# One mask per pair of heads, and VectorE's state scan and output addition placed ahead of the second decay scan

## The chip, the core and the metric

The kernel runs on one core of a Trainium2 chip. The metric is the device time of one launch in microseconds, the median of the runs. The engines named here are TensorE (PE in the profile, its weight loads PEld), VectorE (DVE), ScalarE (ACT), Pool (POOL) and SyncE (SP), which issues the loads. Each works through its own queue in order; semaphores tie the queues together.

## What is computed

Attention with a decaying state, then two mixtures of experts. Only the first part is touched by the change:

```python
def _attn_ref(r, k, v, w, u):             # r, k, v, w: 4 x 8 x 768 x 48
    state = np.zeros((B, H, D, D))
    for t in range(S):
        kt, vt, rt, wt = (k[:, :, t], v[:, :, t], r[:, :, t], w[:, :, t])
        cur = np.einsum('bhd,bhe->bhde', u[None] * kt, vt)
        y[:, :, t] = np.einsum('bhd,bhde->bhe', rt, state + cur)
        state = wt[:, :, :, None] * state + np.einsum('bhd,bhe->bhde', kt, vt)
```

Its output, 3072 rows of 384, goes through a top-1 mixture of 8 experts (`moe_`) with a skip gate, and that result through a second one with slots (`moe2_`).

## The kernel before

The attention runs over 16 pairs of heads (`PAIRS`), two heads side by side in the 128 partitions. A pair's 768 steps are cut into 6 chunks (`NC`) of 128 columns (`C`). Inside a chunk the recurrence becomes a product of scaled inputs: r and k are multiplied by running products of w counted from the middle of the chunk, their scores are masked to earlier steps, and only the states between chunks are carried.

The queues of one pair n, in their order:

- VectorE: `mid_up` (L1215), a scan over half of w; `products`: a reciprocal (L1221), `mid_w` (L1222, five numbers per partition, what each chunk leaves of the state) and the second scan (L1226, `mid_down`); `x_out(n - 3)` (L1260), which adds output and bonus of an earlier pair and frees the output bank `y_cols`; `k_input(n)` (L1240); `chain(n - 1)` (L1253), the scan that carries the states from the chunk sums in PSUM; `r_inputs(n)`: the r product (L1244) and `rk` (L1247).
- TensorE: transposes of k (L543, the fifth chunk at L546), first group of scores `a_products(n, 0)` (L572, two chunks of both heads), bonus rows (L554), second and third group of scores, transposes of the output of pair n - 2 (L605), transposes of the bonus rows (L561), chunk sums (L581), and the output products of pair n - 1 (L593 from the state, L598 from the masked scores).
- ScalarE: spreads `mid_w` over the columns (L1033), copies the output (L999), k (L991, L993), the first scores (L1016), the bonus rows (L1004), the second and third scores, the bonus (L1008), and multiplies v by it in 12 small instructions (`weigh_v`, L1026).
- Pool: three masks (L1586), one per group of scores, 512 columns each, as soon as ScalarE has copied the group.
- SyncE: loads of w, r, k and v, three pairs ahead (L430 to L441).

What ties them: the transposes of k wait for `k_input(n)` and for `chain(n - 1)` (L541); the first scores for the r product; `chain(n)` for the chunk sums of n (L1250) and for the spread middle weights; the output products for the state, for the output bank freed by `x_out` (L589), and for the masks (L595). A group of scores waits for the copy of the group two before it, since there are two buffers. The bonus rows lie in `a_bank`, beside the scores (L345).

Of the kernel before, what the change touches and what calls it, by code (L numbers as in the profile page):

```python
# [11 lines left out]
ACT = mybir.ActivationFunctionType  # L12


def build(nc, wrk, vt, ublock, sizes, w_skip, w_gate, w1, w2, phi, e1, e2, out):
    B, H, S, D = sizes
    P = 128
# [29 lines left out]
    with ctx:  # L47
# [294 lines left out]
        WHOLE = HALF  # L342
        y_cols = y_bank[:, :, :].rearrange("p b t -> p (b t)")[:, 0:S]

        def bonus_cols(g):  # L345

            return a_bank[:, 2 * (g % 2), 2 * C:4 * C]


        def half_rows(t, h0, h1, backwards):  # L350
# [179 lines left out]
        def _(pe):  # L530
# [15 lines left out]
                nc.tensor.transpose(sums_bank[:, NC * D:NC * D + C], k_in[:, c * C:(c + 1) * C], ident[:, :]).then_inc(ktok_full, 1)  # L546

            def bonus_rows(n):
                out = bonus_cols(3 * n + 1)
                if n:  # L550
                    pe.wait_ge(a_copied, 3 * n)
                for c in range(NC):
                    i = c % 4
                    last = nc.tensor.matmul(out[32 * i:32 * i + 32, c // 4 * C:(c // 4 + 1) * C], u_sb[:, n % QP, :], rk[:, c * C:(c + 1) * C],  # L554
                                            start=True, stop=True, tile_position=(0, 32 * i), skip_group_check=True)
                last.then_inc(bonus_full, 1)
# [7 lines left out]
            def a_products(n, s):  # L564
                g = 3 * n + s
                if g >= 2:
                    pe.wait_ge(a_copied, g - 1)
                for c in (2 * s, 2 * s + 1):
                    cols = slice(c * C, (c + 1) * C)
                    for a in range(2):  # L570
                        rows = slice(64 * a, 64 * a + 64)
                        last = nc.tensor.matmul(a_bank[:, 2 * (g % 2) + a, (c % 2) * C:(c % 2 + 1) * C], k_in[rows, cols], r_in[n % 3][rows, cols],  # L572
                                                start=True, stop=True, tile_position=(64 * a, 0), skip_group_check=True)
                last.then_inc(a_full, 1)
# [11 lines left out]
            def y_products(n):  # L586
                pe.wait_ge(state_ready, n + 1)
                if n:
                    pe.wait_ge(y_free, n)  # L589
                for c in range(1, NC):  # L590
                    for a in range(2):
                        rows = slice(64 * a, 64 * a + 64)
                        nc.tensor.matmul(y_cols[64 * a:64 * a + D, c * C:(c + 1) * C], state[n % 2][rows, :, c - 1], r_in[n % 3][rows, c * C:(c + 1) * C],  # L593
                                         start=(c in (1, 4)), stop=False, tile_position=(64 * a, 64 * a), skip_group_check=True)
                pe.wait_ge(a_masked, 3 * n + 3)  # L595
                for c in range(NC):
                    for a in range(2):
                        last = nc.tensor.matmul(y_cols[64 * a:64 * a + D, c * C:(c + 1) * C], v_sb[n % 4][:, c, a, :], a_sb[n % 2][:, a, c, :],  # L598
                                                start=False, stop=True, tile_position=(0, 64 * a), skip_group_check=True)
                last.then_inc(y_full, 1)  # L600

            def y_transposes(n):
                pe.wait_ge(y_copied, n + 1)
                for c in range(NC):
                    last = nc.tensor.transpose(y_cols[:, c * C:(c + 1) * C], y_ch[:, c * C:(c + 1) * C], ident[:, :])  # L605
                last.then_inc(y_turned, 1)
# [5 lines left out]
            for n in range(PAIRS):  # L612
                k_transposes(n)
                pe.wait_ge(r_ready, n + 1)
                a_products(n, 0)
                pe.wait_ge(rk_ready, n + 1)
                bonus_rows(n)
                a_products(n, 1)
                a_products(n, 2)
                if n >= 2:  # L620
                    y_transposes(n - 2)
                pe.wait_ge(ktok_copied, 2 * n + 1)
                bonus_turned(n)
                chunk_sums(n)
                if n:
                    y_products(n - 1)

# [358 lines left out]
        def _(act):  # L986
# [13 lines left out]

            def copy_bonus_rows(n):
                act.wait_ge(bonus_full, 2 * n + 1)
                act.wait_ge(a_full, 3 * n + 2)
                nc.scalar.activation(bonus_ch, bonus_cols(3 * n + 1), ACT.Copy).then_inc(bonus_copied, 1)  # L1004

            def copy_bonus(n):
                act.wait_ge(bonus_full, 2 * n + 2)
# [26 lines left out]
                                     ACT.Copy).then_inc(mid_rows_ready, 1)  # L1034

            act.wait_ge(tables_begun, 2)
            for t, n in ((sums_bank[:, :], 4 * P), (a_bank[:, 0, 2 * C:], 2 * P), (a_bank[:, 2, 2 * C:], 2 * P), (y_cols, S)):
                last = nc.scalar.activation(t, ones_at[:, 0:n], ACT.Copy, scale=0.0)
            last.then_inc(dummy_clear, 1)
            act.wait_ge(tables_begun, 3)  # L1040
            act.sem_inc(y_parts_ready, 1)
            act.sem_inc(h_ready, 1)
            for n in range(PAIRS):
                spread_mid_w(n)
                if n >= 2:
                    copy_y(n - 2)
                copy_ktok(n)
                copy_a(n, 0)
                copy_bonus_rows(n)
                copy_a(n, 1)  # L1050
                copy_a(n, 2)
                copy_bonus(n)
                weigh_v(n)

# [150 lines left out]
        def _(dve):  # L1205
# [9 lines left out]
                V.tensor_tensor_scan(decay[:, 0:SCAN], wrk_sb[i][:, 0:SCAN], ones_at[:, :], 0.0, ALU.mult, ALU.add).then_inc(mid_up_ready, 1)  # L1215

            def products(n):
                i = n % 3
                rows = decay[:, :].rearrange("p (g m) -> p g m", m=ROW)
                dve.wait_ge(mid_up_ready, n + 1)  # L1220
                V.reciprocal(inv_at[:, :].rearrange("p (g m) -> p g m", m=ROW)[:, :, 0], rows[:, 0:2 * NC, WHOLE]).then_inc(inv_ready, 1)  # L1221
                V.tensor_tensor(mid_w[n % 2][:, :], rows[:, NC:2 * NC - 1, WHOLE], rows[:, 1:NC, WHOLE], ALU.mult).then_inc(mid_w_ready, 1)  # L1222
                dve.wait_ge(inv_ready, n + 1)
                if n == 0:
                    dve.wait_ge(ld_small, 16)
                V.tensor_tensor_scan(decay[:, SCAN:2 * SCAN], wrk_sb[i][:, SCAN:2 * SCAN], inv_at[:, :], 0.0,  # L1226
                                     ALU.mult, ALU.add).then_inc(mid_down_ready, 1)
# [42 lines left out]
            dve.wait_ge(tables_begun, 3)  # L1270
            mid_up(0)
            products(0)
            k_input(0)
            r_inputs(0)
            for n in range(1, PAIRS):
                mid_up(n)
                products(n)
                if n >= 3:
                    x_out(n - 3)
                k_input(n)  # L1280
                chain(n - 1)
                r_inputs(n)

            def gate_copies(q):
# [268 lines left out]
        def _(pool):  # L1553
# [26 lines left out]
            nc.gpsimd.iota(name[:, :], pattern=[[1, NT]], base=-NOWHERE, channel_multiplier=LINE, **kw).then_inc(tables_ready, 1)  # L1580

            for n in range(PAIRS):
                for s in range(3):
                    pool.wait_ge(a_copied, 3 * n + s + 1)
                    x = a_sb[n % 2][:, :, 2 * s:2 * s + 2, :]
                    nc.gpsimd.affine_select(out=x, in_=x, compare_op=ALU.is_gt, fill=0.0, base=0,  # L1586
                                            pattern=[[0, 2], [0, 2], [1, C]], channel_multiplier=-1).then_inc(a_masked, 1)

            pool.sem_inc(weight_there, 1)
            pool.sem_inc(stage_turned, 1)  # L1590
# [173 lines left out]
```

## Time and profile before

| | |
|---|---|
| median of 3 runs | 387.31 us (386.09, 387.31, 389.81) |
| profiled execution, span | 387.5 us |
| busy over the span | PE 354.1, DVE 281.8, ACT 221.0, POOL 115.0 us |
| attention, pairs 3 to 15 | a pair every 8.10 us |
| first transposes of k | 9.3 us; those of the last pair at 130.7 us |

The profile is of one execution; its span, 387.5 us, stands 0.2 us above the median of the runs. Timeline rows give the start from the beginning of the span, the duration, the engine, the line of the kernel, the operation and the tiles (output <- inputs); xN says how many instructions are merged, and a bracket at the end the idle time ahead of the row and what ended it. A float32 product counts twice in xN. The recorded duration of an instruction reaches past the start of the next by the pipeline's depth, so steps from start to start are used where instructions follow one another.

### The profile page before, as it was taken

What the parts mean: (1) busy time and instruction counts of PE and PEld (TensorE: products, weight loads), DVE (VectorE), ACT (ScalarE), POOL (GpSimd) and SP (SyncE); (2) the same over time, 40 slices, a digit from 0 to 9 for tenths busy, and PEclk for the clock granted to TensorE, in tenths of its full rate; (3) what the DMA queues carried; (4) which work ended last, traced back from release to release, by engine and by line L of the source; (5) the groups of instructions that cost most, each with busy time, mean ns of one, the idle gap of its engine ahead of it and who ended that gap; (6) DMA issues with size and microseconds to landing.
All of it is one profiled execution on the core that took longest, in us unless ns stands there. A gap on an engine that the chain in (4) does not pass through costs nothing.

```text
span 387.5 us, 14814 instructions
## 1 busy us (share of the span) xinstructions
PE 354.1 (91%) x5880; PEld 269.6 (70%) x5880; DVE 281.8 (73%) x564; ACT 221.0 (57%) x681; POOL 115.0 (30%) x179
## 2 busy tenths in 40 slices
PE   6699999999999999889999999999999999679990
PEld 6487777877777788656777777777777777345360
DVE  7999999999999634786676767777677776430371
ACT  3777888778887755134656556565555664200060
POOL 3543322343223340254222233332221224540000
PEclk9989999999999999989999999999999999689996
DMA  8987656766568995013193799495858779759438
GB/s 310 415 305 265 241 198 216 257 258 248 197 205 286 424 402 205 3 23 111 29 393 128 300 323 393 178 361 193 325 211 321 263 259 396 281 170 327 167 152 336
DMA packets 31300, 97.58 MB, mean 252 GB/s; under 512 B 4062, under 2 KB 14410, under 8 KB 29722
## 3 DMA queue, kind: packets, MB, share of 16 engines
q1 hardware_dynamic: 29466, 93.81, 65.2%
q0 software_dynamic: 1792, 3.17, 2.7%
q8 instruction: 31, 0.51, 0.5%
q14 instruction: 11, 0.09, 0.1%
HBM read 85.53 MB, written 11.45 MB: 250 GB/s over the span
## 4 chain that ended last, share of the span: by engine, by line
PE 56%; DVE 5%; another core or an unknown queue 3%; issue 1%; POOL 1%; ACT 1%; DVEq 0%; ACTq 0%
PE a_bank L772 19%; PE y_bank L781 18%; PE y_bank L928 3%; PE a_bank L944 3%; PE a_bank L637 2%; DVE x_all L1550 2%; PE sums_bank L705 1%; PE a_bank L832 1%; PE y_bank L598 1%; PE y_bank L593 1%; PE ktok_bank L645 1%; PE sums_bank L645 1%; PE y_bank L605 1%; PE y_bank L740 0%
## 5 line engine op out<-in xcount | busy, mean ns | idle before, releaser
L781 PE MATMUL y_bank<-w_sb,work 128*32 128x192 f32 x1664 | 78.5, 326 | 0.5 <-ACT work L1131 0.5
L772 PE MATMUL a_bank<-w_sb,work 128*32 128x256 f32 x1248 | 77.9, 382 | 0.1
L781 PEld LDWEIGHTS y_bank<-w_sb,work 128*32 128x32 f32 x1664 | 64.9, 110 | 8.8 <-DVE work L1396 1.1
L1586 POOL TENSOR_SCALAR_AFFINE_SELECT a_sb<-a_sb 128x512 f32<-128x512 f32 x48 | 44.2, 932 | 86.7 <-ACT a_sb L1016 86.7
L772 PEld LDWEIGHTS a_bank<-w_sb,work 128*32 128x32 f32 x1248 | 42.4, 109 | 25.6 <-issue 13.0
L1026 ACT ACTIVATE bonus_v<-v_sb,bonus 128x48 f32<-128x48 f32 x192 | 45.0, 321 | 14.0 <-DVE x_all L1260 13.9
L1104 ACT ACTIVATE work<-work 32x96 f32<-32x96 f32 x108 | 30.4, 281 | 39.3 <-PE a_bank L772 37.0
L1440 DVE TENSOR_TENSOR ys<-work 32x192 f32<-32x192 f32 x104 | 37.0, 355 | 9.9 <-ACT work L1131 9.2
L1396 DVE STREAM_TRANSPOSE work<-hid 128x256 f32<-128x256 f32 x53 | 23.6, 446 | 26.2 <-PE y_bank L781 22.9
L572 PE MATMUL a_bank<-r_in,k_in 64*128 64x128 f32 x384 | 31.0, 295 | 0.1
L572 PEld LDWEIGHTS a_bank<-r_in,k_in 64*128 64x128 f32 x384 | 24.7, 193 | 6.3 <-issue 5.7
L1215 DVE TENSOR_TENSOR_SCAN decay<-wrk_sb,ones_at 128x780 f32<-128x780 f32 x16 | 28.3, 1771 | 0.8 <-DMA wrk_sb<-in_wrk 0.8
L1226 DVE TENSOR_TENSOR_SCAN decay<-wrk_sb,inv_at 128x780 f32<-128x780 f32 x16 | 28.3, 1770 | 0.0
L1391 DVE COPY work<-work 32x96 f32<-32x96 f32 x108 | 26.5, 246 | 2.4 <-PE a_bank L772 0.2
L593 PE MATMUL y_bank<-r_in,state 64*48 64x128 f32 x320 | 21.4, 276 | 7.5 <-DVE x_all L1260 7.4
L1130 ACT ACTIVATE work<-y_bank 64x192 f32<-64x192 f32 x52 | 16.8, 324 | 17.8 <-PE y_bank L781 17.8
L1016 ACT ACTIVATE a_sb<-a_bank 128x512 f32<-128x512 f32 x48 | 26.8, 595 | 0.1
L1659 POOL COPY weight_i<-put_i 128x1 uint32 x13 | 2.4, 181 | 75.9 <-DVE x_all L1413 75.9
L593 PEld LDWEIGHTS y_bank<-r_in,state 64*48 64x48 f32 x320 | 18.3, 159 | 9.1 <-issue 9.0
L598 PE MATMUL y_bank<-a_sb,v_sb 128*48 128x128 f32 x384 | 24.3, 276 | 0.0
L598 PEld LDWEIGHTS y_bank<-a_sb,v_sb 128*48 128x48 f32 x384 | 20.2, 123 | 2.4
L1110 ACT ACTIVATE hid<-a_bank 128x256 f32<-128x256 f32 x53 | 20.3, 383 | 2.7 <-PE a_bank L772 1.4
(314 smaller groups left out, 582.6 us busy)
## 6 DMA issues: line engine op xcount, KB each, us to landing
w_sb<-in_moe_w SPq DMA_DIRECT2D x20, 1536.0 KB, 11.7
wrk_sb<-in_wrk SPq DMA_DIRECT2D x16, 768.0 KB, 7.0
e_sb<-in_moe_w SPq DMA_DIRECT2D x8, 1536.0 KB, 11.0
wrk_sb<-in_wrk SPq DMA_DIRECT2D x15, 780.0 KB
v_sb<-in_vt SPq DMA_DIRECT2D x16, 288.0 KB, 2.9
tokens<-x_all SPq DMA_DIRECT2D x4, 1152.0 KB, 21.7
out<-x_all SPq DMA_DIRECT2D x12, 384.0 KB, 3.9
x_all<-in_moe_w SPq DMA_DIRECT2D x2, 1536.0 KB
```

What stands on the lines that cost most here:

```text
L572: last = nc.tensor.matmul(a_bank[:, 2 * (g % 2) + a, (c % 2) * C:(c % 2 + 1) * C], k_in[rows, cols], r_in[n % 3][rows, cols], start=True, ...
L593: nc.tensor.matmul(y_cols[64 * a:64 * a + D, c * C:(c + 1) * C], state[n % 2][rows, :, c - 1], r_in[n % 3][rows, c * C:(c + 1) * C], start ...
L598: last = nc.tensor.matmul(y_cols[64 * a:64 * a + D, c * C:(c + 1) * C], v_sb[n % 4][:, c, a, :], a_sb[n % 2][:, a, c, :], start=False, sto ...
L772: last = nc.tensor.matmul(out[SUB * g:SUB * (g + 1), 0:FB], x[:, kk, :], w1_sb[j][:, kk, FB * g:FB * (g + 1)], start=(kk == 0), stop=(kk = ...
L781: last = nc.tensor.matmul(bank[4][SUB * g:SUB * (g + 1), 0:YW], h_t[:, SUB * k:SUB * (k + 1)], w2_sb[j][:, k, d:d + YW], start=(b == 0), s ...
L1016: nc.scalar.activation(a_sb[n % 2][:, :, 2 * s:2 * s + 2, :].rearrange("p a c t -> p a (c t)"), a_bank[:, 2 * (g % 2):2 * (g % 2) + 2, 0:2 ...
L1026: last = nc.scalar.activation(bonus_v[n % 2][:, c, a, :], v_sb[n % 4][:, c, a, :], ACT.Copy, scale=bonus[:, c, a:a + 1])
L1104: last = nc.scalar.activation(x[SUB * o:SUB * (o + 1), :, :], turned[SUB * s:SUB * (s + 1), :].rearrange("p (k o t) -> p k o t", o=PER, t= ...
L1215: V.tensor_tensor_scan(decay[:, 0:SCAN], wrk_sb[i][:, 0:SCAN], ones_at[:, :], 0.0, ALU.mult, ALU.add).then_inc(mid_up_ready, 1)
L1226: V.tensor_tensor_scan(decay[:, SCAN:2 * SCAN], wrk_sb[i][:, SCAN:2 * SCAN], inv_at[:, :], 0.0, ALU.mult, ALU.add).then_inc(mid_down_ready, 1)
L1440: last = V.tensor_tensor(ys[SUB * s:SUB * (s + 1), YW * d:YW * (d + 1)], y_low[rows, :], y_high[rows, :], ALU.add)
L1586: nc.gpsimd.affine_select(out=x, in_=x, compare_op=ALU.is_gt, fill=0.0, base=0, pattern=[[0, 2], [0, 2], [1, C]], channel_multiplier=-1).t ...
```

## The change

- Pool makes one mask over all six chunks of a pair, after the third copy of scores and (but for the last pair) after the `mid_w` of the next pair. The output products wait for one mask per pair.
- On VectorE the second scan becomes `mid_down`, and the order is now `mid_up`, `products`, `x_out(n - 3)`, `chain(n - 1)`, `mid_down(n)`, `k_input(n)`, `r_inputs(n)`. Before, it was `mid_up`, `products` with that scan, `x_out`, `k_input`, `chain`, `r_inputs`.
- On TensorE: first and second scores, output transposes, third scores, bonus rows, chunk sums, bonus transposes, output products. The bonus rows are written to `ktok_bank` once the transposed k is copied out of it.
- On ScalarE the middle weights are spread one pair ahead, between the copy of the bonus rows and that of the bonus; the three copies of scores follow one another. Two clears of the old place of the bonus rows fall away.

```diff
-        def bonus_cols(g):
-            return a_bank[:, 2 * (g % 2), 2 * C:4 * C]
+        bonus_cols = ktok_bank[:, 2 * C:4 * C]
...
             def bonus_rows(n):
-                out = bonus_cols(3 * n + 1)
-                if n:
-                    pe.wait_ge(a_copied, 3 * n)
+                pe.wait_ge(ktok_copied, 2 * n + 1)
+                out = bonus_cols
...
-                pe.wait_ge(a_masked, 3 * n + 3)
+                pe.wait_ge(a_masked, n + 1)
...
                 a_products(n, 0)
+                a_products(n, 1)
+                if n >= 2:
+                    y_transposes(n - 2)
+                a_products(n, 2)
                 pe.wait_ge(rk_ready, n + 1)
                 bonus_rows(n)
-                a_products(n, 1)
-                a_products(n, 2)
-                if n >= 2:
-                    y_transposes(n - 2)
-                pe.wait_ge(ktok_copied, 2 * n + 1)
+                chunk_sums(n)
                 bonus_turned(n)
-                chunk_sums(n)
                 if n:
                     y_products(n - 1)
...
             def copy_bonus_rows(n):
                 act.wait_ge(bonus_full, 2 * n + 1)
-                act.wait_ge(a_full, 3 * n + 2)
-                nc.scalar.activation(bonus_ch, bonus_cols(3 * n + 1), ACT.Copy).then_inc(bonus_copied, 1)
+                nc.scalar.activation(bonus_ch, bonus_cols, ACT.Copy).then_inc(bonus_copied, 1)
...
+            spread_mid_w(0)
             for n in range(PAIRS):
-                spread_mid_w(n)
                 if n >= 2:
                     copy_y(n - 2)
                 copy_ktok(n)
                 copy_a(n, 0)
-                copy_bonus_rows(n)
                 copy_a(n, 1)
                 copy_a(n, 2)
+                copy_bonus_rows(n)
+                if n < PAIRS - 1:
+                    spread_mid_w(n + 1)
                 copy_bonus(n)
                 weigh_v(n)
...
                 V.tensor_tensor(mid_w[n % 2][:, :], rows[:, NC:2 * NC - 1, WHOLE], rows[:, 1:NC, WHOLE], ALU.mult).then_inc(mid_w_ready, 1)
+
+            def mid_down(n):
+                i = n % 3
                 dve.wait_ge(inv_ready, n + 1)
...
                 products(n)
                 if n >= 3:
                     x_out(n - 3)
+                chain(n - 1)
+                mid_down(n)
                 k_input(n)
-                chain(n - 1)
                 r_inputs(n)
...
             for n in range(PAIRS):
-                for s in range(3):
-                    pool.wait_ge(a_copied, 3 * n + s + 1)
-                    x = a_sb[n % 2][:, :, 2 * s:2 * s + 2, :]
-                    nc.gpsimd.affine_select(out=x, in_=x, compare_op=ALU.is_gt, fill=0.0, base=0,
-                                            pattern=[[0, 2], [0, 2], [1, C]], channel_multiplier=-1).then_inc(a_masked, 1)
+                pool.wait_ge(a_copied, 3 * n + 3)
+                if n < PAIRS - 1:
+                    pool.wait_ge(mid_w_ready, n + 2)
+                x = a_sb[n % 2][:, :, :, :]
+                nc.gpsimd.affine_select(out=x, in_=x, compare_op=ALU.is_gt, fill=0.0, base=0,
+                                        pattern=[[0, 2], [0, NC], [1, C]], channel_multiplier=-1).then_inc(a_masked, 1)
```

## Rows read from the trace of the kernel before

**Rows 1.** The page: the span, and the clock granted to TensorE in 40 slices.

```profile
span 387.5 us, 14814 instructions
PEclk9989999999999999989999999999999999689996
```

**Rows 2.** One pair by stage: window, length, busy us of each engine, clock, DMA share, GB/s.

```profile
74.10:82.20 8.10, 7.52 (x116) 6.31 (x114) 8.06 (x10) 6.47 (x23) 2.60 (x3) 1.00 0.62 234
```

**Rows 3.** Timeline, VectorE in one pair: start us, duration us, instruction.

```profile
74.69 1.77 DVE L1215 TENSOR_TENSOR_SCAN decay<-wrk_sb,ones_at 128x780 f32<-128x780 f32 x1
76.87 1.77 DVE L1226 TENSOR_TENSOR_SCAN decay<-wrk_sb,inv_at 128x780 f32<-128x780 f32 x1
78.56 0.72 DVE L1260 TENSOR_TENSOR x_all<-y_bank,bonus_v 128x576 f32<-128x576 f32 x1
79.21 1.27 DVE L1240 TENSOR_TENSOR k_in<-wrk_sb,decay 128x768 f32<-128x768 f32 x1
80.40 0.74 DVE L1253 TENSOR_TENSOR_SCAN state<-sums_bank,mid_rows 128x288 f32<-128x288 f32 x1
81.07 0.93 DVE L1244 TENSOR_TENSOR r_in<-wrk_sb,decay 128x768 f32<-128x768 f32 x1
81.92 0.94 DVE L1247 TENSOR_TENSOR work<-wrk_sb 128x768 f32<-128x768 f32 x1
```

**Rows 4.** Timeline, TensorE in the same pair, and the last pair's first row.

```profile
74.05 0.66 PE L543 MATMUL ktok_bank<-ident,k_in 128*128 128x128 f32 x4
74.74 0.71 PE L572 MATMUL a_bank<-r_in,k_in 64*128 64x128 f32 x8
75.39 0.63 PE L554 MATMUL a_bank<-work,u_sb 128*32 128x128 f32 x12
75.94 1.16 PE L572 MATMUL a_bank<-r_in,k_in 64*128 64x128 f32 x16
77.04 0.88 PE L605 MATMUL y_bank<-ident,batch_t 128*128 128x128 f32 x6
77.75 0.38 PE L561 MATMUL ktok_bank<-ident,batch_t 128*128 128x128 f32 x2
78.06 0.79 PE L581 MATMUL sums_bank<-v_sb,k_tok 128*64 128x48 f32 x20
79.43 1.34 PE L593 MATMUL y_bank<-r_in,state 64*48 64x128 f32 x20 [0.58 <-DVE x_all L1260]
...
130.74 0.66 PE L543 MATMUL ktok_bank<-ident,k_in 128*128 128x128 f32 x4
```

**Rows 5.** Waits from 30 to 130 us: waiter <- releaser: total us, times, longest.

```profile
PE y_bank L593 <- DVE x_all L1260: 7.4, 13, 0.6
```

**Rows 6.** Timeline, Pool: a 128-column select, one pair's three masks, the last two masks.

```profile
1.26 0.29 POOL L1556 TENSOR_SCALAR_AFFINE_SELECT ident<-ident 128x128 f32<-128x128 f32 x1 [0.25 <-POOL ident L1554]
...
76.29 0.64 POOL L1586 TENSOR_SCALAR_AFFINE_SELECT a_sb<-a_sb 128x512 f32<-128x512 f32 x1 [4.72 <-ACT a_sb L1016]
77.71 1.36 POOL L1586 TENSOR_SCALAR_AFFINE_SELECT a_sb<-a_sb 128x512 f32<-128x512 f32 x1 [0.78 <-ACT a_sb L1016]
79.03 0.63 POOL L1586 TENSOR_SCALAR_AFFINE_SELECT a_sb<-a_sb 128x512 f32<-128x512 f32 x1
...
134.41 1.23 POOL L1586 TENSOR_SCALAR_AFFINE_SELECT a_sb<-a_sb 128x512 f32<-128x512 f32 x2 [0.78 <-ACT a_sb L1016]
```

**Rows 7.** Timeline of the first two pairs, VectorE and TensorE.

```profile
8.23 0.96 DVE L1240 TENSOR_TENSOR k_in<-wrk_sb,decay 128x768 f32<-128x768 f32 x1 [0.41 <-DMA wrk_sb<-in_wrk]
...
13.26 1.77 DVE L1226 TENSOR_TENSOR_SCAN decay<-wrk_sb,inv_at 128x780 f32<-128x780 f32 x1
...
15.12 1.16 DVE L1240 TENSOR_TENSOR k_in<-wrk_sb,decay 128x768 f32<-128x768 f32 x1
...
17.09 0.63 PE L543 MATMUL ktok_bank<-ident,k_in 128*128 128x128 f32 x4 [3.06 <-DVE state L1253]
```

**Rows 8.** Timeline, ScalarE: the copy of one group of scores, same pair.

```profile
75.64 0.58 ACT L1016 ACTIVATE a_sb<-a_bank 128x512 f32<-128x512 f32 x1
```

More of the change, by code:

```diff
@@ L1036, in _ @@
             act.wait_ge(tables_begun, 2)
-            for t, n in ((sums_bank[:, :], 4 * P), (a_bank[:, 0, 2 * C:], 2 * P), (a_bank[:, 2, 2 * C:], 2 * P), (y_cols, S)):
+            for t, n in ((sums_bank[:, :], 4 * P), (y_cols, S)):
                 last = nc.scalar.activation(t, ones_at[:, 0:n], ACT.Copy, scale=0.0)
@@ L1217, in products @@
             def products(n):
-                i = n % 3
                 rows = decay[:, :].rearrange("p (g m) -> p g m", m=ROW)
@@ L1272, in _ @@
             products(0)
+            mid_down(0)
             k_input(0)
```

## The prediction, made before the result was known

> **What bounds the kernel now.** I read the page first: one execution of 387.5 us, TensorE granted its upper clock level (2.4 GHz) in nearly all slices [rows 1]. The diff touches only the attention stage, the first 138 us or so: 16 pairs of heads. So the next view was the busy time by stage inside one pair. A pair takes 8.10 us, and VectorE is busy for 8.06 of them, TensorE for 7.52, ScalarE for 6.47, Pool for 2.60 [rows 2]. VectorE is the bound of a pair, with TensorE half a microsecond behind.
>
> The timeline of VectorE shows the order: `mid_up` scan, two small instructions, `mid_down` scan, output addition, `k_input`, state scan (`chain`), `r_inputs`, and the next `mid_up` follows without a hole [rows 3]. TensorE's timeline shows the other side: from the transposes of k at 74.05 to the end of the chunk sums at 78.85 (78.06 + 0.79) it works without a stop, then it stands 0.58 us until the output addition has freed the output bank [rows 4]; 13 such waits make 7.4 us [rows 5]. TensorE runs behind VectorE: nothing that VectorE needs from it comes late.
>
> Pool's masks have a price on VectorE. The third mask of a pair ends at 79.66; `k_input` began at 79.21 and took 1.27 us [rows 3, 6], where the same instruction alone took 0.96 [rows 7]. It lost 0.31 us: it moved only from 79.52 on, 0.14 before the mask's recorded end. The second mask took 1.36 instead of 0.64: it started under the `mid_down` scan and finished 0.43 after it [rows 3, 6]. The two last masks took 1.23 together although the output addition ran beside them, so that instruction costs them nothing [rows 6]. Instructions with both operands in SBUF (the scans over `wrk_sb`, `k_input`) and masks exclude each other; the output addition and the state scan, with one operand in PSUM, do not.
>
> **The change, part by part.** I follow one pair n from K, the end of its `k_input`, and ask when the next `k_input` can end.
>
> *Masks.* Three per pair become one of 1536 columns. A 128-column select took 0.29 and a 512-column one 0.64 [rows 6], so 0.0009 us a column, and the large one is 0.64 + 1024 x 0.0009 = 1.56 us. The upper bound is three small ones, 3 x 0.64 = 1.91. For the lower one, the stopped mask still needed 0.43 behind the scan's end, so three times that and 0.1 for a start, 1.4. Placed beside output addition and state scan it no longer meets `k_input`: 0.31 off VectorE, whose own work falls to 8.10 - 0.31 = 7.79 us a pair. It would be a gain if VectorE stayed the bound (rival 2).
>
> *The state scan goes ahead of `mid_down` and `k_input`.* This is the part that decides. Before, the state scan of pair n stood behind `k_input` of pair n+1; the scan waits for pair n's chunk sums on TensorE, and TensorE's pair n+1 waits for `k_input`. Now the waits form a ring: `k_input`(n), then `r_inputs`, scores, chunk sums (n), state scan (n), `mid_down`(n+1), `k_input`(n+1). No work of VectorE can fill the wait for the sums, since `mid_down`, `k_input` and `r_inputs` are queued behind the waiting scan, and TensorE waits for those. The ring, step by step:
>
> - r product: starts 0.08 before K (80.40 against 80.48), takes 0.93, ends K + 0.85 [rows 3]. One hand-off of 0.07, which is what copy to mask takes (76.22 to 76.29) [rows 6, 8]: first scores at K + 0.92. TensorE is ready before: transposes to scores is 74.74 - 74.05 = 0.69 [rows 4].
> - First and second scores: as the two groups of before, 75.94 to 77.04, 1.10. Output transposes: 0.60 from first to last start and 0.20 to the next kind, 0.80; their step to the bonus transposes was 0.71, because nothing changed shape there, while each change of the tile's shape costs 0.20 instead of 0.11 [rows 4]. Third scores 0.65 (as 74.74 to 75.39), bonus rows 0.55 (75.39 to 75.94), chunk sums 0.79 to their end. Together 3.89: sums end at K + 4.81. The bonus transposes are taken out of the way, 0.31; the shape changes once more than before.
> - State scan at K + 4.88 (hand-off), the next instruction 0.67 later (80.40 to 81.07) [rows 3]: `mid_down` at K + 5.55.
> - `mid_down` to `k_input`: 1.86, since `k_input` needs the scan's result (13.26 to 15.12) [rows 7]. With the output addition between them this latency was hidden and the step was 1.69 (76.87 to 78.56) [rows 3]. `k_input` 0.96. The ring closes at K + 8.37.
>
> The Trainium skill, VectorE: DVE Perf Modes, section on the DRAIN, says that a semaphore between VectorE instructions costs nothing extra; by it the step would be 1.69 and the ring 8.20. The trace disagrees with 1.86, and I keep the row.
>
> VectorE meanwhile is ready for the state scan at K - 0.08 + 1.72 (r product and `rk`, 81.07 on, to the next pair's scan at 74.69 + 8.10) + 2.1 (that scan and the small ones, 2.18 before with a mask in the way) + 0.65 (output addition) = K + 4.4 [rows 3], and then idles about half a microsecond. The output transposes are done by K + 3.0, so the addition itself is not late.
>
> *Where the large mask falls.* It needs the copy of the third scores. These end at K + 0.92 + 1.10 + 0.80 + 0.71 = 3.53; hand-off and copy 0.07 + 0.58 [rows 8], hand-off 0.07: mask from K + 4.25 to 5.81, and it frees the operand path 0.14 before its end, at 5.67. `mid_down`, ready at 5.55, waits until then: 0.12 more. The ring becomes 8.49. The wait for the middle weights (K + 3.8) is over by then.
>
> The Trainium skill, GPSIMD Engine Reference, sections Specifications and Engine selection, puts Pool at 1.2 GHz and a one-input instruction near one element a cycle; the 1024 further columns would then take 0.85, the mask 1.49, the ring 8.42, an estimate from that page. The 512-column row needs no such rate, and I stay with the slope of two rows.
>
> *Middle weights a pair ahead, bonus rows later.* ScalarE has 6.47 of 8.10 busy; its spreading (0.39) moves to a place after the bonus copy, and `weigh_v` no longer waits for the addition. The bonus copy ends near K + 4.6, before the sums end, so the transposes behind them don't wait. Cost nothing, covered by 0.5 us or more of idle in each pair. TensorE's output products now find their bank free: its 0.58 wait goes, and a wait for `k_input` takes its place. SP's loads are asked for three pairs ahead; no step of them moves past another.
>
> **The sum.** Between pair 3 and pair 15 lie 12 periods: 12 x (8.49 - 8.10) = 4.7 us. The first pairs: `k_input`(0) ends at 9.19. The same walk, with the third scores held until the first copy frees its bank, brings the sums to 13.5 and the mask to 13.2 to 14.8 (behind the middle weights); `mid_down`(1), at 13.26 before, starts at 14.64, and `k_input`(1) ends at 17.46 against 16.28 before [rows 7]. Pair 1 has no output transposes, ring 7.6, but TensorE, idle for 3 us before 17.09 then and longer now, works part of it at the lower clock level of 1.2 GHz (the third slice, from 19.4 to 29.1 us, shows 0.8, so 0.2 of it or more went at half speed [rows 1]). VectorE's own work hid that, the ring doesn't: about 1.3 if most of some 3 us at half speed is TensorE's work, and 0 to 1.7 as bounds. `k_input`(2) ends near 26.4, `k_input`(3) at 34.9, pair 3's transposes start at 35.0. Before they started at 130.74 - 12 x 8.10 = 33.54 [rows 4]: +1.5. Behind pair 15 the walk from scores to output products is 4.18 in both orders, and the later stages are reached through TensorE, so they shift whole. Total 4.7 + 1.5 = 6.2 on the profiled 387.5: 393.7. The median of the three runs, 387.31, is 0.2 below that execution; I predict 393.4.
>
> **Rivals.**
> 1. *The ring without the mask's hold* (mask near 1.4, or copies a little earlier): ring 8.37, 12 x 0.27 = 3.2, start 0.9: 391.4. Speaks for it: the margin is 0.12 us. Chance 0.25. If hand-offs are 0.05 too, 390.8.
> 2. *Faster: VectorE stays the bound.* Its own queue gives 4.4 + 0.67 + 1.86 + 0.96 = 7.9 a pair, or 7.8 if the small product is freed wholly: 12 x 0.3 = 3.6 less, 383.7. It decides when the sums end before VectorE is ready for the state scan; TensorE would have to be 0.4 to 0.5 quicker over 3.9 us than rows 4 make it. For it speaks only that the 0.31 on `k_input` is surely saved. Chance 0.05.
> 3. *No semaphore latency*, the page's rule above: ring 8.20 or 8.32 with the hold, 12 x 0.22 + 1.3: 391.2. Chance 0.05, as the trace has 1.86 in its rows.
> 4. *A slower mask*, 1.7 to 1.91: the hold grows to 0.26 to 0.47, 12 x 0.25 and a start of 0.3 more: 395.5 to 398. Chance 0.15.
> 5. *The mask comes after `mid_down`* has started, is stopped by it and then holds `k_input` for 1.4: 12 x 1.4, over 405. It has 1.3 us of room. Chance 0.02.
>
> The forecast itself has 0.48. The range takes rival 1 and most of rival 4: 389.8 to 396.8. Runs of this kernel lie 3.7 us apart, so about 1% (3.9 us) is what can be told from no change. Slower by more than that (over 391.2): the forecast, rivals 4 and 5, and a third of rival 1, 0.74. Faster by more (under 383.4): most of rival 2, 0.04. Within: the rest, 0.22.
>
> **What would show it.** Right: a pair of 8.4 to 8.5 us; VectorE with some half microsecond idle ahead of the state scan, released by the chunk sums, and TensorE idle before the transposes of k, released by `k_input`; `k_input` at 0.96; one mask of about 1.56 per pair, starting under the state scan's wait; a `mid_down` recorded a little over 1.77. Wrong: VectorE without a hole and a pair under 8.1 (rival 2), `mid_down` at 1.77 with the mask gone before it (rival 1), or a mask of 3 us that ends under `k_input` (rival 5). The weakest numbers are the slope of the mask, the 0.07 of each hand-off, and the low clock at the start.

## The result

Timed together with the kernel before, four runs each: 395.25 us (393.44 to 395.98) after, 388.56 (386.09 to 390.04) before, ratio 1.0176 with an interval of 1.0123 to 1.0228. Timed again on chip 8 (`e9_changed_again` below) the ratio is 1.0188, 1.0174 to 1.0202. The changed kernel is 1.8% slower. The forecast was 393.4, from 389.8 to 396.8, and slower. Of the 1.9 us between 393.4 and 395.25, 1.25 lie in the kernel before, whose median rose from 387.31 to 388.56 with its fourth run, and 0.6 in the difference of the two kernels (6.7 against 6.1).

One pair of the changed kernel by stage, which answers to [rows 2]: a pair now takes 8.48 us, TensorE busy 7.74, VectorE 7.88 of them.

```profile
76.80:85.28 8.48, 7.74 (x117) 6.26 (x113) 7.88 (x10) 6.79 (x23) 1.55 (x1) 1.00 0.64 224
```

VectorE's timeline of one pair (answers to [rows 3]; K, the end of `k_input`, is 77.51):

```profile
76.55 0.96 DVE L1239 TENSOR_TENSOR k_in<-wrk_sb,decay 128x768 f32<-128x768 f32 x1
77.43 0.95 DVE L1243 TENSOR_TENSOR r_in<-wrk_sb,decay 128x768 f32<-128x768 f32 x1
78.30 0.95 DVE L1246 TENSOR_TENSOR work<-wrk_sb 128x768 f32<-128x768 f32 x1
79.17 1.78 DVE L1212 TENSOR_TENSOR_SCAN decay<-wrk_sb,ones_at 128x780 f32<-128x780 f32 x1
81.12 0.10 DVE L1218 TENSOR_TENSOR mid_w<-decay 128x5 f32<-128x5 f32 x1
81.14 0.75 DVE L1259 TENSOR_TENSOR x_all<-y_bank,bonus_v 128x576 f32<-128x576 f32 x1
82.37 0.76 DVE L1252 TENSOR_TENSOR_SCAN state<-sums_bank,mid_rows 128x288 f32<-128x288 f32 x1 [0.48 <-PE sums_bank L578]
83.04 1.90 DVE L1225 TENSOR_TENSOR_SCAN decay<-wrk_sb,inv_at 128x780 f32<-128x780 f32 x1
85.03 0.96 DVE L1239 TENSOR_TENSOR k_in<-wrk_sb,decay 128x768 f32<-128x768 f32 x1
```

The order is the new one. `k_input` is back at 0.96 and the small product `mid_w` at 0.10 (0.31 before, at 76.64), so masks meet neither. But there is a hole that [rows 3] did not have: after the output addition VectorE stands 0.48 us until the chunk sums are there. And the second decay scan is recorded at 1.90 instead of 1.77.

TensorE in the same pair (answers to [rows 4]), then the waits from 30 to 130 us (answers to [rows 5]):

```profile
77.57 0.66 PE L541 MATMUL ktok_bank<-ident,k_in 128*128 128x128 f32 x4 [0.64 <-DVE k_in L1239]
78.43 1.16 PE L569 MATMUL a_bank<-r_in,k_in 64*128 64x128 f32 x16
79.53 0.87 PE L602 MATMUL y_bank<-ident,batch_t 128*128 128x128 f32 x6
80.33 0.71 PE L569 MATMUL a_bank<-r_in,k_in 64*128 64x128 f32 x8
80.97 0.63 PE L551 MATMUL ktok_bank<-work,u_sb 128*32 128x128 f32 x12
81.53 0.79 PE L578 MATMUL sums_bank<-v_sb,k_tok 128*64 128x48 f32 x20
...
82.62 1.34 PE L590 MATMUL y_bank<-r_in,state 64*48 64x128 f32 x20
```

```profile
PEld ktok_bank L541 <- DVE k_in L1239: 10.7, 12, 0.9
...
PE ktok_bank L541 <- DVE k_in L1239: 7.7, 12, 0.6
DVE state L1252 <- PE sums_bank L578: 5.8, 12, 0.5
```

TensorE's wait for the output addition is gone, and one for `k_input` is there instead, 0.64 us a pair. Two engines each waiting for the other, once a pair: that is the ring. Pool's timeline shows its second part, the one mask (answers to [rows 6]):

```profile
81.76 1.55 POOL L1588 TENSOR_SCALAR_AFFINE_SELECT a_sb<-a_sb 128x1536 f32<-128x1536 f32 x1 [6.92 <-ACT a_sb L1011]
```

It ends at 83.31, the second scan was asked for at 83.04; the scan's 1.90 is 0.13 more than it needs.

The last pair's transposes of k start at 136.91 us against 130.74 before [rows 4]. That is 6.2 us. The profiled spans differ by 5.4 only (392.9 and 387.5): the rest of the kernel, which the change doesn't touch, was 0.8 us shorter in this execution. Behind the attention, the granted clock of the 40 slices differs in one place:

```profile
PEclk9899999999999999989999999999999999979996
```

Before [rows 1], TensorE was granted 0.6 and 0.8 of the full clock in slices 35 and 36; after, 0.9 and 0.7. The stretch around it, from the last expert products of the first mixture to the second mixture's products back, took 44.6 us before and 42.0 after; the stretches on either side were 1.4 and 0.4 us longer after. Such differences between executions are in the medians of four runs too, which are 6.7 apart.

### The profile page after: what moved, and what is told of

Its sections match the earlier page's. It is cut to its first block, busy times and chain, and to the rows that moved or that the text cites. A ratio compares the mean times of both kernels' runs of the same rounds, so it can differ in the third digit from the quotient of the medians.

```text
span 392.9 us, 14764 instructions
## 1 busy us (share of the span) xinstructions
PE 358.3 (91%) x5880; PEld 274.0 (70%) x5880; DVE 278.9 (71%) x564; ACT 225.0 (57%) x679; POOL 96.1 (24%) x147
## 4 chain that ended last, share of the span: by engine, by line
PE 54%; DVE 7%; another core or an unknown queue 1%; issue 1%; DVEq 0%; ACT 0%; ACTq 0%
PE a_bank L768 19%; PE y_bank L777 18%; PE y_bank L924 3%; PE a_bank L940 3%; PE a_bank L633 2%; PE a_bank L701 2%; DVE x_all L1551 1%; PE a_bank L828 1%; PE y_bank L595 1%; PE y_bank L590 1%; PE ktok_bank L641 1%; PE sums_bank L641 1%; PE y_bank L602 1%; DVE batch_t L1358 1%
## 5 line engine op out<-in xcount | busy, mean ns | idle before, releaser
L777 PE MATMUL y_bank<-w_sb,work 128*32 128x192 f32 x1664 | 79.8, 326 | 0.6 <-ACT work L1128 0.5
L768 PE MATMUL a_bank<-w_sb,work 128*32 128x256 f32 x1248 | 79.1, 382 | 0.2
L777 PEld LDWEIGHTS y_bank<-w_sb,work 128*32 128x32 f32 x1664 | 66.3, 110 | 8.5 <-DVE work L1397 1.2
L768 PEld LDWEIGHTS a_bank<-w_sb,work 128*32 128x32 f32 x1248 | 43.5, 109 | 25.2 <-issue 12.5
L1588 POOL TENSOR_SCALAR_AFFINE_SELECT a_sb<-a_sb 128x1536 f32<-128x1536 f32 x16 | 24.8, 1550 | 113.1 <-ACT a_sb L1011 104.4
L1225 DVE TENSOR_TENSOR_SCAN decay<-wrk_sb,inv_at 128x780 f32<-128x780 f32 x16 | 30.3, 1894 | 0.0
L541 PE MATMUL ktok_bank<-ident,k_in 128*128 128x128 f32 x64 | 10.9, 296 | 13.5 <-DVE k_in L1239 13.5
## 6 DMA issues: line engine op xcount, KB each, us to landing
w_sb<-in_moe_w SPq DMA_DIRECT2D x20, 1536.0 KB, 11.7
```

The source lines that it names most:

```text
L768: last = nc.tensor.matmul(out[SUB * g:SUB * (g + 1), 0:FB], x[:, kk, :], w1_sb[j][:, kk, FB * g:FB * (g + 1)], start=(kk == 0), stop=(kk = ...
L777: last = nc.tensor.matmul(bank[4][SUB * g:SUB * (g + 1), 0:YW], h_t[:, SUB * k:SUB * (k + 1)], w2_sb[j][:, k, d:d + YW], start=(b == 0), s ...
```

## The experiments

All are judged first by the profile of the loop over the pairs, then by the time. A pair is the mean distance of `k_input` over pairs 8 to 14. In most runs each pair repeats to 0.01 us; in `e4_mid_down_first` and `e10_first_again` the transposes of k start 7.68 and 7.72 us apart in turn, in `e8_tensor_as_before` 7.68 and 7.86. Three theories were to be told apart: the ring (my forecast), the large mask as the cause, and TensorE's new order as the cause.

### Each part of the change alone

`e1_vector_order`, the kernel before with VectorE's order alone:

```diff
-                k_input(n)
                 chain(n - 1)
+                mid_down(n)
+                k_input(n)
                 r_inputs(n)
```

> The kernel before with VectorE's new order alone (output addition, state scan, then the second decay scan and k_input); TensorE's order, ScalarE's order and the three masks are those of before. Ring theory: the wait for the chunk sums alone makes a pair longer. TensorE's old order is worse for it, since the bonus rows wait for rk and the bonus transposes stand ahead of the sums: sums end near K + 5.2, state scan 5.3, second scan 5.95, k_input ends at 8.8 us. A pair of 8.75 to 8.85 us, VectorE idle ahead of the state scan. Time 395 to 398 us. Rival, the large mask is what costs: a pair of 8.1 or less, since no large mask is there and the third mask no longer meets k_input (about 7.9). Rival, TensorE's new order is what costs: also 8.1 or less.

Measured: a pair of 8.78 us, 401.56 us in one run beside 390.13 before; the last pair's transposes start at 142.42, 11.7 us late. VectorE's timeline:

```profile
85.30 0.76 DVE L1263 TENSOR_TENSOR x_all<-y_bank,bonus_v 128x576 f32<-128x576 f32 x1 [0.54 <-PE y_bank L605]
86.18 0.76 DVE L1256 TENSOR_TENSOR_SCAN state<-sums_bank,mid_rows 128x288 f32<-128x288 f32 x1
86.85 1.76 DVE L1229 TENSOR_TENSOR_SCAN decay<-wrk_sb,inv_at 128x780 f32<-128x780 f32 x1
88.70 0.96 DVE L1243 TENSOR_TENSOR k_in<-wrk_sb,decay 128x768 f32<-128x768 f32 x1
```

TensorE's chunk sums in the same pair:

```profile
85.34 0.79 PE L581 MATMUL sums_bank<-v_sb,k_tok 128*64 128x48 f32 x20
```

So VectorE's order alone makes the kernel slower, and more than the whole change does. The length of a pair was met; the place of the hole was not. VectorE waits 0.54 us ahead of the output addition, for the output transposes, which in TensorE's old order come late, and then 0.2 more ahead of the state scan. The ring closes through the sums all the same: they end at 86.13 and the state scan starts at 86.18, which is K + 5.30 (K = 80.88), where 5.3 was expected. Without the wait for the transposes VectorE would have stood there longer. The time, of one run, is 11.4 us above the kernel before on the same chip (390.13) and outside the 395 to 398 that I had expected: 12 x 0.68 = 8.2, and 3.5 in the first pairs.

`e2_one_mask`, the kernel before with the one mask alone (Pool's loop and the wait for it as in the change):

> The kernel before with one mask a pair alone. Ring theory: no ring here, VectorE stays the bound and the state scan is not waited for. The mask wakes after the third copy, under the second decay scan, is stopped until that scan ends, then runs 1.4 us, beside the output addition first and into k_input: k_input grows from 1.27 to about 1.60 us, while the small product mid_w falls to 0.10. A pair of 8.3 to 8.4 us, so the large mask in the old order costs as well, but by another way. Rival, the large mask is the whole cause of the slower kernel: a pair of 8.48 or more. If masks didn't stop VectorE at all: 7.8.

Measured: a pair of 8.32 us, 389.92 us in one run. VectorE's and Pool's timelines:

```profile
87.40 0.10 DVE L1222 TENSOR_TENSOR mid_w<-decay 128x5 f32<-128x5 f32 x1
...
89.22 0.73 DVE L1260 TENSOR_TENSOR x_all<-y_bank,bonus_v 128x576 f32<-128x576 f32 x1
89.87 1.59 DVE L1240 TENSOR_TENSOR k_in<-wrk_sb,decay 128x768 f32<-128x768 f32 x1
```

```profile
88.65 2.00 POOL L1587 TENSOR_SCALAR_AFFINE_SELECT a_sb<-a_sb 128x1536 f32<-128x1536 f32 x1 [6.32 <-ACT a_sb L1016]
```

As expected to the hundredth: `mid_w` at 0.10, `k_input` at 1.60. The mask was stopped by the scan that began at 87.53, ran beside the output addition and then held `k_input`. In the old order one large mask costs 0.22 us a pair; it is not what makes 8.48. The last pair's transposes start at 134.43, 3.7 us later than before, which the one time doesn't show: the stages behind them were 3.1 us shorter in this execution (253.7 against 256.8), as they differ from one execution to the next.

`e3_three_masks`, the changed kernel with the three masks of before:

> The changed kernel with the three masks of before, each as soon as its copy is there; all orders stay changed. Ring theory: only the hold of the second decay scan goes. Its third mask ends near K + 5.0 and frees the operands before the scan starts; the ring closes at 8.36 instead of 8.48, the second scan is recorded at 1.77 to 1.78 instead of 1.90, VectorE still waits about 0.4 to 0.5 us for the chunk sums. Time about 391 us. Rival, the large mask is the cause: a pair of 8.1 or less and no wait.

Measured: a pair of 8.34, 392.03 us in one run. VectorE's timeline:

```profile
88.78 0.28 DVE L1218 TENSOR_TENSOR mid_w<-decay 128x5 f32<-128x5 f32 x1
...
90.03 0.76 DVE L1252 TENSOR_TENSOR_SCAN state<-sums_bank,mid_rows 128x288 f32<-128x288 f32 x1 [0.31 <-PE sums_bank L578]
90.71 1.76 DVE L1225 TENSOR_TENSOR_SCAN decay<-wrk_sb,inv_at 128x780 f32<-128x780 f32 x1
```

The second decay scan is at 1.76 again. The wait for the sums stays, 0.31 us after a `mid_w` that the masks now lengthen to 0.28. So the mask's share in the slower pair is 8.48 - 8.34 = 0.14, and 0.24 over the 8.10 of before remains without any large mask.

`e5_vector_as_before`, the changed kernel with VectorE's order put back; one mask, TensorE's and ScalarE's new orders:

```diff
                 products(n)
+                mid_down(n)
                 if n >= 3:
                     x_out(n - 3)
-                chain(n - 1)
-                mid_down(n)
                 k_input(n)
+                chain(n - 1)
                 r_inputs(n)
```

> The changed kernel with VectorE's order put back to that of before; one mask, TensorE's and ScalarE's new orders stay. Ring theory: no ring, VectorE is the bound again, and the one mask meets k_input as it did when it alone was put into the kernel before: a pair of 8.32 us, k_input 1.60, no wait for the chunk sums. So TensorE's and ScalarE's new orders are worth nothing by themselves here. Rival, TensorE's new order is the cause of the slower kernel: a pair near 8.48.

Measured: a pair of 8.32 us; 384.97 us in one run, on a chip where the kernel before takes 379.73. One row:

```profile
90.04 1.59 DVE L1239 TENSOR_TENSOR k_in<-wrk_sb,decay 128x768 f32<-128x768 f32 x1
```

The same pair as in `e2_one_mask`, 8.32 and 1.59, and the last pair's transposes at 134.57 (134.43 there). With VectorE's old order, TensorE's and ScalarE's new orders neither cost nor gain anything: the third theory falls. With VectorE's new order they gain: from `e1_vector_order` to `e3_three_masks`, which differ in them and in the place of the bonus rows alone, a pair falls from 8.78 to 8.34.

### Two paths of the ring

`e6_sums_first`, the changed kernel with the chunk sums ahead of the bonus rows:

```diff
+                chunk_sums(n)
                 pe.wait_ge(rk_ready, n + 1)
                 bonus_rows(n)
-                chunk_sums(n)
                 bonus_turned(n)
```

> The changed kernel with the chunk sums ahead of the bonus rows on TensorE, so the sums end 0.56 us earlier. The third scores, their copy and the mask stay where they are. If the mask's hold and the sums are two paths of nearly the same length, as read: the state scan starts at K + 4.3, its wait for the sums falls from 0.48 us to nearly nothing, the second decay scan starts 0.56 earlier and is stopped by the mask until K + 5.67 all the same: it is recorded at about 2.45 us, and a pair stays at 8.48. If the mask's hold is a small extra and only the sums bind, a pair falls to about 7.95.

Measured: a pair of 8.48, unchanged; 388.26 us beside 379.73. VectorE and Pool:

```profile
89.83 0.75 DVE L1259 TENSOR_TENSOR x_all<-y_bank,bonus_v 128x576 f32<-128x576 f32 x1
90.51 0.76 DVE L1252 TENSOR_TENSOR_SCAN state<-sums_bank,mid_rows 128x288 f32<-128x288 f32 x1
91.18 2.46 DVE L1225 TENSOR_TENSOR_SCAN decay<-wrk_sb,inv_at 128x780 f32<-128x780 f32 x1
93.73 0.96 DVE L1239 TENSOR_TENSOR k_in<-wrk_sb,decay 128x768 f32<-128x768 f32 x1
```

```profile
90.45 1.55 POOL L1588 TENSOR_SCALAR_AFFINE_SELECT a_sb<-a_sb 128x1536 f32<-128x1536 f32 x1 [6.93 <-ACT a_sb L1011]
```

The state scan follows the addition without a wait. The scan behind it is asked for at 91.18, 0.56 us earlier in the pair than in the changed kernel, and takes 2.46: it stands until the mask, ending at 92.00, lets go. The whole gain of 0.56 is given back there. In the changed kernel two paths of nearly equal length lead around the ring, one over the sums (8.34 by itself, as `e3_three_masks` has it) and one over the third copy and the mask (8.48); `e3_three_masks` takes the second away, `e6_sums_first` the first, and each alone brings little or nothing. Both at once with the rest unchanged was not run.

### The latency between a scan and what needs it

`e7_product_between`, the changed kernel with the r times k product moved:

```diff
                 mid_down(n)
+                rk_product(n)
                 k_input(n)
                 r_inputs(n)      # without that product
```

> The changed kernel with the r times k product (0.95 us, 0.87 from start to start) moved from behind the r product to between the second decay scan and k_input; it needs nothing of the scan. It prices the latency from the scan to the instruction that needs its result. If that latency is real (1.86 from start to start with nothing between, against 1.69 when another stands between), the step from scan to k_input is 1.69 + 0.87 = 2.56 plus the mask's hold, and a pair grows by 0.70 to about 9.2. If the wait costs nothing extra, as the page's rule has it, the step grows by the full 0.87 and a pair is about 9.35.

Measured: a pair of 9.15 us; 398.57 us beside 379.73. VectorE:

```profile
88.61 0.76 DVE L1256 TENSOR_TENSOR_SCAN state<-sums_bank,mid_rows 128x288 f32<-128x288 f32 x1 [1.11 <-PE sums_bank L578]
89.28 1.90 DVE L1225 TENSOR_TENSOR_SCAN decay<-wrk_sb,inv_at 128x780 f32<-128x780 f32 x1
91.10 0.93 DVE L1233 TENSOR_TENSOR work<-wrk_sb 128x768 f32<-128x768 f32 x1
91.95 0.94 DVE L1246 TENSOR_TENSOR k_in<-wrk_sb,decay 128x768 f32<-128x768 f32 x1
```

Scan to product is 1.82, less the hold of 0.13 that is 1.69; product to `k_input` 0.85. The pair grew by 0.67 and not by 0.87: the instruction between hides the latency. The first decay scan, which waits for the r product that now stands directly ahead of it, starts 1.03 us behind it (83.67 to 84.70), where the step from the r product to the next instruction was 0.87. The step of 1.86 is real, and 0.17 us of it is latency: nearly half of the 0.38 that a pair lost.

### One move that frees the ring

`e4_mid_down_first`, the changed kernel with the second decay scan back ahead of the output addition; the state scan still stands ahead of `k_input`:

```diff
                 products(n)
+                mid_down(n)
                 if n >= 3:
                     x_out(n - 3)
                 chain(n - 1)
-                mid_down(n)
                 k_input(n)
                 r_inputs(n)
```

> The changed kernel with one move: the second decay scan goes back ahead of the output addition and the state scan; those two still stand ahead of k_input, and the mask is still one. Ring theory: the second scan (1.7 us) now fills the time in which the sums are made. The sums come before VectorE asks for them, the ring is 4.8 + 0.07 + 0.67 + 0.9 = 6.4 us and no longer binds, and the latency from the second scan to k_input is hidden again. The mask wakes under the second scan, is stopped by it, and runs beside output addition and state scan (1.32 us) for its 1.4 us, so k_input is held by 0.1 at most. TensorE's own 7.65 us and VectorE's 7.7 to 7.8 bind: a pair of 7.7 to 7.85 us, 12 x 0.3 to 0.4 less than before, 382 to 384 us, faster than both. Rival, the cost lies in the large mask: a pair of 8.3 to 8.5 as in the changed kernel. Rival, the cost lies in TensorE's new order: 8.4.

Measured: a pair of 7.70 us; 383.44 us (six runs) beside 390.13, ratio 0.9846, 0.9801 to 0.9891. Faster than both. VectorE, Pool, and the busy time from 30 to 120 us:

```profile
84.38 0.73 DVE L1259 TENSOR_TENSOR x_all<-y_bank,bonus_v 128x576 f32<-128x576 f32 x1
85.03 0.74 DVE L1252 TENSOR_TENSOR_SCAN state<-sums_bank,mid_rows 128x288 f32<-128x288 f32 x1
85.69 0.94 DVE L1239 TENSOR_TENSOR k_in<-wrk_sb,decay 128x768 f32<-128x768 f32 x1
...
90.37 1.78 DVE L1225 TENSOR_TENSOR_SCAN decay<-wrk_sb,inv_at 128x780 f32<-128x780 f32 x1
92.07 0.73 DVE L1259 TENSOR_TENSOR x_all<-y_bank,bonus_v 128x576 f32<-128x576 f32 x1
```

```profile
84.27 1.55 POOL L1588 TENSOR_SCALAR_AFFINE_SELECT a_sb<-a_sb 128x1536 f32<-128x1536 f32 x1 [6.13 <-ACT a_sb L1011]
```

```profile
30.00:120.00 90.00, 89.60 (x1330) 73.57 (x1324) 89.44 (x106) 76.98 (x249) 18.64 (x12) 1.00 0.68 247
```

No hole on VectorE, none on TensorE: 89.4 and 89.6 us of 90 busy. `k_input` takes 0.94. The mask starts at 84.27, as soon as the third copy ends (84.21), and has the output addition and the state scan beside it, 84.38 to 85.69. That the second scan would stop it, as I had expected, is not in these rows: that scan is recorded to 84.46 and the mask took its 1.55. The chunk sums end at 84.84, 0.19 before the state scan starts at 85.03: VectorE doesn't wait for them.

`e8_tensor_as_before`: the same relief with fewer edits. The kernel before, with one mask, and one line moved:

```diff
                 if n >= 3:
                     x_out(n - 3)
-                k_input(n)
                 chain(n - 1)
+                k_input(n)
                 r_inputs(n)
```

> The kernel before with only two edits: one mask a pair, and k_input behind output addition and state scan (the second decay scan stays ahead of them). TensorE's and ScalarE's orders are those of before. Ring theory: the same relief as with all orders changed; the second scan fills the time in which the sums are made and stops the mask until it can run beside the two instructions with an operand in PSUM. A pair of 7.7 to 7.75 us, time 382 to 385, faster than before by 1.2 to 1.8%. If TensorE's new order was needed for it, 8.0 or more.

Measured: a pair of 7.77 us, 376.93 (six runs) beside 379.73, ratio 0.9922, 0.9903 to 0.9940. VectorE:

```profile
86.12 0.73 DVE L1260 TENSOR_TENSOR x_all<-y_bank,bonus_v 128x576 f32<-128x576 f32 x1
86.89 0.76 DVE L1253 TENSOR_TENSOR_SCAN state<-sums_bank,mid_rows 128x288 f32<-128x288 f32 x1
87.57 0.99 DVE L1240 TENSOR_TENSOR k_in<-wrk_sb,decay 128x768 f32<-128x768 f32 x1
```

The pair is 0.07 us longer than with all orders changed (I had expected 7.70 to 7.75) and 0.33 shorter than before. In this pair the sums end at 86.85 and the state scan starts at 86.89, 0.1 later than the addition would let it; in the next pair it doesn't wait. So the sums still come a little late in every second pair. The time fell by 0.8% where I had expected 1.2 to 1.8. Its last transposes start at 128.65, 2.1 us earlier than before, not the 4.0 that 12 x 0.33 give: pair 3's transposes stood 1.9 us later than in the profile of the kernel before. `k_input` of the first pair ended at 9.91 instead of 9.19 [rows 7], which is 0.7 of it and waited for a load; it varies between executions of one program (9.25 in `e4_mid_down_first`, 9.74 in `e10_first_again`). What this order costs in the first pairs was not taken apart further.

Last, the changed kernel and `e4_mid_down_first` timed together on one chip:

> The changed kernel unaltered, timed together with the version of the next run on one chip. From the pair periods: 12 x 0.38 and 1.6 in the first pairs, 6.2 us slower than before, ratio 1.016.

Measured: 387.14 us beside 380.30, ratio 1.0188 (1.0174 to 1.0202); a pair of 8.48, last transposes at 136.90.

> The changed kernel with the second decay scan ahead of output addition and state scan, again, beside the changed kernel on the same chip. A pair of 7.70 us as in its first profile; 4.3 us before the last pair's transposes against the kernel before, 10.4 against the changed one: ratio to before 0.985 to 0.990.

Measured: 376.05 us beside 380.30, ratio 0.9888 (0.9873 to 0.9903); a pair of 7.70, last transposes at 126.51. The two versions differ by one moved scan and by 11.1 us.

| kernel | order on VectorE behind `mid_w` | masks | us a pair |
|---|---|---|---|
| before | mid_down, x_out, k_input, chain | 3 | 8.10 |
| e2 | the same | 1 | 8.32 |
| e5, new TensorE order | the same | 1 | 8.32 |
| e1 | x_out, chain, mid_down, k_input | 3 | 8.78 |
| e3, new TensorE order | the same | 3 | 8.34 |
| changed kernel | the same | 1 | 8.48 |
| e6, sums ahead of bonus rows | the same | 1 | 8.48 |
| e7 | x_out, chain, mid_down, r times k, k_input | 1 | 9.15 |
| e8 | mid_down, x_out, chain, k_input | 1 | 7.77 |
| e4, new TensorE order | the same | 1 | 7.70 |

## Why the prediction was right

*Who binds before.* VectorE, 8.06 of 8.10. Held by `e4_mid_down_first`: once the mask meets neither `mid_w` nor `k_input`, 0.4 us a pair come back.

*The ring.* Its steps against the changed kernel's rows, from K = 77.51: scores at 78.43, K + 0.92 (forecast 0.92); sums end at 82.32, K + 4.81 (4.81); state scan K + 4.86 (4.88); second scan K + 5.53 (5.55); next `k_input` ends K + 8.48 (8.49). Hole ahead of the state scan 0.48 ("about half a microsecond").

*The mask.* 1.55 us (1.56), K + 4.25 to 5.80 (4.25 to 5.81). The slope from two sizes was right. Its hold was 0.13 (0.12), and `e3_three_masks` gives 0.14 for taking it away.

*The latency.* 1.86, kept against the rule of the Trainium skill, VectorE: DVE Perf Modes, section on the DRAIN, that a semaphore costs nothing extra. `e3_three_masks` has 1.85 from scan to `k_input` (90.71 to 92.56), and `e7_product_between` shows it hidden. The measurement decides against the rule for a scan and the product that waits for it; whether the hand-off or the pipeline makes the 0.17 us, no run tells apart.

*The sum.* The 12 periods brought 4.5 us (4.7); the first pairs 1.6, with pair 3's transposes at 35.18 (35.0; 1.5). Together 6.2 at the last pair, as forecast; 6.7 by the medians. That the 6.2 came out exactly is luck in part: 0.4 of the 1.6 is that the first `k_input` ended at 9.58 and not at 9.19, and it varies so from execution to execution (9.24 in `e9_changed_again`, with pair 3 at 35.13).

*The low clock at the start.* Pair 1 ran at a granted clock of 0.81:

```profile
17.70:26.70 9.00, 8.32 (x108) 6.91 (x108) 7.25 (x9) 6.48 (x21) 1.55 (x1) 0.81 0.83 328
```

Its transposes stand 8.96 us before pair 2's (7.6 + 1.3 = 8.9 was forecast); from pair 2 on the clock is at 1.00 and the step 8.48. A mean of 0.81 over 9.0 us is some 3.4 us at half speed, an estimate from that row, beside the "some 3 us" of the forecast. How much of them lay on the ring's path was guessed between 0 and 1.7, and no run separates it.

*What was off.* I set the span of the profiled execution, 387.5, against the median of the times, 387.31, as if both measured the same. A run's time is some 1.8 us longer than its span (394.67 against 392.9 in the changed kernel's profiled run), so "0.2 below" was no statement on that execution. It cost nothing, because the shift was added to both. The untouched stages were taken to shift whole; they came out 0.8 us shorter, for no reason in the change. Two chances were added up loosely: rival 2's 383.7 is not under the 383.4 that it was counted in, and rival 1's 391.4 lies above 391.2, so that more than a third of it counts as slower.

*The rivals.* Rival 1, no hold, is refuted by the 1.90 and by `e3_three_masks`. Rival 2, VectorE stays the bound, needed the sums before VectorE asks. In the changed kernel they came 0.48 us too late for it, but `e4_mid_down_first` reaches it by asking later: its 7.70 is even below the 7.8 to 7.9 that I gave, since there the latency is hidden again. Rival 4, a mask of 1.7 or more, is refuted by the 1.55, and rival 5 by the mask's start at 81.76, 1.28 us before the second scan. What I didn't see is that the fast order lay one moved line away.

## What to carry to other kernels

When an instruction is moved ahead of others in one engine's queue, ask what the instructions behind it feed. Here the state scan waited for TensorE, and the scan and products behind it were what TensorE needed for its next pair: a wait with idle time on both sides, closed to a ring. Put the long work that doesn't depend on the wait ahead of the waiting instruction, and the producers of the other engine's input as early as their own inputs allow; add the steps of such a ring from row to row, latencies of dependent neighbours included.

Saving time on the engine that binds is worth nothing if the new order lets another path bind: 0.31 us of stall on `k_input` were truly removed, and a pair became 0.38 longer.

## What the runs showed of the hardware

- A scan over `wrk_sb` or `k_input`, with both operands in SBUF, that finds a mask on its way goes on 0.13 to 0.14 us before the mask's recorded end, however long it waits: it waited 0.13 us on a scan in the changed kernel, 0.64 on `k_input` in `e2_one_mask`, 0.69 on a scan in `e6_sums_first` (2.46 against 1.77). The output addition and the state scan, with one operand in PSUM, ran beside the mask at 0.73 and 0.74 in `e4_mid_down_first`.
- The stages behind the attention took different times on different chips. From the last expert products of the first mixture to the second mixture's products back, where both kernels have the same code, in the profile of the kernel before and in `e8_tensor_as_before` on chip 5:

```profile
313.00:358.00 45.00, 38.53 (x510) 24.51 (x506) 18.77 (x56) 12.73 (x38) 16.07 (x20) 0.89 0.81 289
```

```profile
311.00:346.00 35.00, 33.70 (x502) 22.25 (x498) 18.48 (x55) 12.65 (x37) 16.16 (x20) 1.00 0.94 350
```

45 us against 35, with 289 and 350 GB/s moved and TensorE's clock at 0.89 and 1.00. The changed kernel's own two profiles have 42.0 us there in the first and 35.0 in `e9_changed_again` on chip 8. The kernel before took 390.13 us on chip 14, 379.73 on chip 5 and 380.30 on chip 8 (on which chip the first timing, with 388.56, ran is not known). It is no difference of kernels; each chip was measured at one time only, so that it is the chip's own is likely and not shown. The loop doesn't show it: a pair of the changed kernel is 8.48 us in both its profiles. Whether the memory or the clock makes it was not tried.
